# A two-layer MLP behind a per-head tap filter: the order of the prologue on VectorE and ScalarE, the taps, the first loads and the fillers between the turns

## The reference

```
# x (2, 4096, 192), weight_gen (2, 4096, 8 heads, 7 taps), all float32
w = exp(weight_gen - max over taps);  w = w / (sum over taps + 1e-9)
x1[s] = sum over k of w[s, head, k] * x_pad[s + k]        # 6 zero rows ahead of the sequence
x2 = relu(x1 @ w_in) ** 2 @ w_out                         # 192 -> 2048 -> 192
h  = x2 @ w_in2;  out = (h * clip(h + 3, 0, 6) / 6) @ w_out2
```

## Time and profile before

| what | value |
|---|---|
| median of the runs shown | 1148.89 us (1148.46 to 1148.95, 3 runs) |
| the profiled execution's own time | 1147.57 us |
| its span | 1145.8 us |
| busy in the span: TensorE, VectorE, ScalarE | 1128.2, 911.6, 667.6 us |
| TensorE waits for the three turns' taps | 9.4 us |
| mean granted clock of TensorE | 0.995 of full |

### The profile page before, as it was taken

One profiled execution on the slowest core, in us unless ns is written; L12 is line 12 of the kernel. 1 busy time (PEld: TensorE's weight loads), 2 busy tenths in 40 slices (PEclk: granted clock), 3 DMA queues, 4 the chain that ended last, 5 costly groups with the idle time before them and its releaser, 6 DMA issues.

```text
span 1145.8 us, 25809 instructions
## 1 busy us (share of the span) xinstructions
PE 1128.2 (98%) x10046; PEld 1058.5 (92%) x10046; DVE 911.6 (80%) x1005; ACT 667.6 (58%) x741; POOL 3.1 (0%) x10
## 2 busy tenths in 40 slices
PE   9889999999999999999999999999999999999998
PEld 8779899999999999999999999999999999999997
DVE  6768888796987969788796987969788796986665
ACT  5758555556556564655556565564555656565554
POOL 1000000000000000000000000000000000000000
PEclk9989999999999999999999999999999999999999
DMA  7302102002020110202002020110302002010011
GB/s 203 80 2 74 35 6 69 12 14 62 4 73 6 52 28 0 76 4 68 12 9 67 4 72 7 43 37 0 76 4 67 13 3 72 0 38 4 1 16 28
DMA packets 79303, 41.29 MB, mean 36 GB/s; under 512 B 56172, under 2 KB 72300, under 8 KB 79272
## 3 DMA queue, kind: packets, MB, share of 16 engines
q1 hardware_dynamic: 79272, 40.86, 13.8%
HBM read 29.42 MB, written 11.40 MB: 36 GB/s over the span
## 4 chain that ended last, share of the span: by engine, by line
PE 94%; DVE 2%; ACT 2%; issue 1%; DMA 0%; SPq 0%; DVEq 0%; ACTq 0%
PE h_ps L965 44%; PE y_ps L976 29%; PE y_ps L985 20%; DVE acc L620 1%; ACT hid L452 1%; ACT hid L447 1%; ACT hid_hi L460 0%; DVE hid_lo L737 0%; DMA outs<-in_x_dram 0%; DVE prod L635 0%; PE y_ps L954 0%; PE h_ps L915 0%; PE h_ps L944 0%; DVE hid L728 0%; PE y_ps L1070 0%
## 5 line engine op out<-in xcount | busy, mean ns | idle before, releaser
L965 PE MATMUL h_ps<-xt,win 64*128 64x512 f32 (+1 forms) x4644 | 1070.5, 384 | 0.0
L965 PEld LDWEIGHTS h_ps<-xt,win 64*128 64x128 f32 x4644 | 844.8, 185 | 30.4 <-DVE wout L703 0.7
L976 PE MATMUL y_ps<-hid_hi,wout 64*128 64x512 f32 (+1 forms) x2064 | 547.0, 384 | 1.4 <-DVE xt L711 1.4
L463 ACT ACTIVATE hid_hi<-hid 128x1024 fp32r<-128x1024 f32 (+1 forms) x242 | 255.2, 1054 | 334.2 <-DVE hid L728 161.0
L737 DVE TENSOR_TENSOR hid_lo<-hid,hid_hi 128x1024 fp32r<-128x1024 f32 (+1 forms) x258 | 311.2, 1206 | 161.0 <-ACT hid_hi L463 142.4
L976 PEld LDWEIGHTS y_ps<-hid_hi,wout 64*128 64x128 f32 x2064 | 377.7, 185 | 15.5 <-DVE xt L711 2.1
L985 PE MATMUL y_ps<-hid_lo,wout 64*128 64x512 f32 (+1 forms) x1032 | 313.7, 384 | 0.0
L985 PE MATMUL y_ps<-hid_hi,wout 64*128 64x512 f32 (+1 forms) x1032 | 313.7, 384 | 0.0
L976 PE MATMUL y_ps<-hid_lo,wout 64*128 64x512 f32 (+1 forms) x1032 | 313.6, 384 | 0.0
L985 PEld LDWEIGHTS y_ps<-hid_hi,wout 64*128 64x128 f32 x1032 | 189.7, 185 | 6.9
L985 PEld LDWEIGHTS y_ps<-hid_lo,wout 64*128 64x128 f32 x1032 | 189.7, 185 | 6.8
(11 more groups left out here) (88 smaller groups left out, 333.6 us busy)
## 6 DMA issues: line engine op xcount, KB each, us to landing
xwin<-in_x_dram SPq DMA_DIRECT2D x14, 960.0 KB, 5.7
by_feature<-stage SPq DMA_DIRECT2D x52, 96.0 KB, 2.0
out_dram<-outs SPq DMA_DIRECT2D x240, 16.0 KB, 1.5
out_dram<-outs SPq DMA_DIRECT2D x240, 8.0 KB, 1.4
stage<-by_feature SPq DMA_DIRECT2D x13, 256.0 KB, 3.1
stage<-in_moe_w_out_dram SPq DMA_DIRECT2D x8, 384.0 KB, 4.8
stage<-in_moe_w_in_dram SPq DMA_DIRECT2D x8, 256.0 KB, 3.8
stage<-in_moe_w_in_dram SPq DMA_DIRECT2D x16, 128.0 KB, 3.3
```

The lines of the kernel that those rows point to most:

```text
L463: act.activation(hi, hid[:, slot, :, 0:width], ACT.Copy).then_inc(hi_done, 1)
L965: return pe.matmul(h_ps[:, s % 2, t, 0:tokens.stop - tokens.start], win[layer][r, wn, cols], src[r, xn, tokens], start=bool(rows) and n in ...
L976: return pe.matmul(ps[:, 0, tokens], wout[layer][r, tile, w_cols], src, start=bool(rows) and s == 0 and n == 0 and half != 1, stop=not row ...
```

## The change

It writes the prologue's order anew; the loop is untouched.

- SP issues only the near rows of the last 15 partitions of each half; ScalarE's queue issues the other near rows (48 partitions each) as its first act.
- TensorE's first matmuls use a square of ones that VectorE sets, instead of the identity from GpSimd: 14 instead of 15. Between the turned products of chunk 0 two matmuls on 64 rows each stand where one on the whole array stood, and 2 instead of 3 close them.
- Taps of chunk 1 and 2 stand a step or more earlier. The half 0 turn stands behind the first body of step 7 instead of ahead of it, and `split_x1` of a half stands in the step before.
- The squares of steps 10 and 11 go from VectorE to ScalarE, that of step 14 from ScalarE to VectorE. Weight piece 5 is copied by ScalarE, piece 10 by VectorE; the pieces are spread anew. For chunk 0 `y_cross` is copied ahead of `y_main`, and VectorE's add needs only the former.
- SP asks for chunk 1's gates and rows after 6 instead of 10 pieces.

```diff
-    OWN_HI = (5, 7)
+    OWN_HI = (7, 10)
-    GATED = range(10, 14)
-    WARM = 15
+    GATED = (12, 13, 14)
+    WARM = 14
+    MOST, FEW = [(1, 49)], [(49, PB)]
@@ SyncE
-            load_halo(HALO // 2, HALO // 2, x_near_loaded)
-            load_halo(0, HALO // 2, x_far_loaded)
-            for n in range(10):
+            load_halo(sp, HALO // 2, HALO // 2, x_near_loaded, FEW)
+            load_halo(sp, 0, HALO // 2, x_far_loaded, MOST + FEW)
+            for n in range(6):
                 load_piece(n)
             sp.wait_ge(exp_done, 1)
             load_gates(1)
             load_rows(J, J, x_second_loaded)
@@ ScalarE
+            load_halo(act, HALO // 2, HALO // 2, x_near_loaded, MOST)
             act.wait_ge(consts_set, 1)
...
-                if g == 7:
-                    split_x1_hi(1, xt[0], y1_ps, 0)
-                if g == 10:
-                    copy_y(0, STEPS, y2_ps)
...
+                if g == 6:
+                    split_x1_hi(1, xt[0], y1_ps, 0)
...
+                if g == 9:
+                    copy_y(0, STEPS, y2_ps)
@@ VectorE
+            dve.memset(ones, 1.0).then_inc(ones_set, 1)
...
-                dve.wait_ge(y_copied, 2 * c + 2)
+                dve.wait_ge(y_copied, 2 * c + (1 if cross_first(c) else 2))
@@ TensorE
-            def identities(count):
+            def multiply(square, count):
+
                 for n in range(count):
-                    pe.matmul(h_ps[:, 0, 0, 0:P], ident[:, :], ident[:, :], start=True, stop=True)
+                    pe.matmul(h_ps[:, 0, 0, 0:P], square, square, start=True, stop=True)
+
+            def fill():
+                for bank, r in enumerate(ROWS_OF):
+                    pe.matmul(h_ps[:, bank, 0, 0:P], ident[r, :], ident[r, :], start=True, stop=True, tile_position=(r.start, 0))
...
+            pe.wait_ge(ones_set, 1)
+            multiply(ones, WARM)
             pe.wait_ge(ident_ready, 2)
-            identities(WARM)
             for m in range(TAPS):
                 turn_product(m)
                 if m >= 2:
-                    identities(1)
-            identities(3)
+                    fill()
+            multiply(ident[:, :], 2)
...
-                if g == STEPS - 1:
-                    pe.wait_ge(prep_done, prep_value(1, f"add{TAPS - 1}", 0))
-                    turn_att(1, y1_ps, 0)
                 if g == STEPS + SPLIT - 1:
                     pe.wait_ge(prep_done, prep_value(1, f"add{TAPS - 1}", 1))
+                    pe.wait_ge(y_copied, 2)
                     pe.wait_ge(y_added, 1)
                     turn_att(1, y2_ps, 1)
...
                 first_body(g, inn, late, g >= SECOND + 2)
+                if g == STEPS - 1:
+                    pe.wait_ge(prep_done, prep_value(1, f"add{TAPS - 1}", 0))
+                    turn_att(1, y1_ps, 0)
```

More of the change, by code:

```diff
@@ L157, in conv_mlp_kernel @@
         products = [acc[:, :], prod[:, 0, :], prod[:, 1, :], free_hid[:, 0:J * D], free_hid[:, J * D:2 * J * D]]
+        ones = y_main[:, 0:P]
         ident = sb("ident", [P, P])
@@ L283, in gated_value, with cross_first @@
         def gated_value(g):
-            if isinstance(g, int) and g < GATED.stop:
-                return g + 1 - GATED.start
+            if isinstance(g, int) and g < SECOND:
+                return sum(n <= g for n in GATED)
             return g + 1 - (SECOND - len(GATED))
+        def cross_first(c):
+            return isinstance(c, int) and c == 0
         def narrow(g):
@@ L293, in squared_value, with load_halo @@
         def squared_value(g):
-            return g + 1 if g < GATED.start else g + 1 - len(GATED)
+            return g + 1 - gated_value(g)
         block = ctx.enter_context(nc.Block())
+        def load_halo(engine, row, rows, loaded, groups):
+            for start, stop in groups:
+                for b in range(B):
+                    source = bass.AP(x.tensor, ((b * PB + start) * ROWS + row - HALO) * D,
+                                     [[ROWS * D, stop - start], [1, rows * D]])
+                    engine.dma_start(xwin_first[b * PB + start:b * PB + stop, row * D:(row + rows) * D], source).then_inc(loaded, 16)
         @block.sync
@@ L306, in load_piece @@
                     sp.dma_start(dst, src).then_inc(piece_loaded[n], 16)
-            def load_halo(row, rows, loaded):
-                for start, stop in ((1, EVEN), (EVEN, PB)):
-                    for b in range(B):
-                        source = bass.AP(x.tensor, ((b * PB + start) * ROWS + row - HALO) * D,
-                                         [[ROWS * D, stop - start], [1, rows * D]])
-                        sp.dma_start(xwin_first[b * PB + start:b * PB + stop, row * D:(row + rows) * D], source).then_inc(loaded, 16)
             def load_rows(row, rows, loaded):
@@ L383, in _ @@
             load_rows(J, J, x_second_loaded)
-            for n in range(10, PIECES + 3):
+            for n in range(6, PIECES + 1):
                 load_piece(n)
@@ L388, in _ @@
             load_window(2)
-            for n in range(PIECES + 3, 2 * PIECES - 1):
+            for n in range(PIECES + 1, 2 * PIECES):
                 load_piece(n)
@@ L489, in copy_y @@
                     act.wait_ge(x2_lo, 2 * c)
-                act.activation(y_main[:, :], ps[:, 0, :], ACT.Copy).then_inc(y_copied, 1)
-                act.activation(y_cross[:, :], ps[REST:P, 1, :], ACT.Copy).then_inc(y_copied, 1)
+                parts = [(y_main, ps[:, 0, :]), (y_cross, ps[REST:P, 1, :])]
+                for dst, src in parts[::-1] if cross_first(c) else parts:
+                    act.activation(dst[:, :], src, ACT.Copy).then_inc(y_copied, 1)
             def split_x2_main_hi(c, dst):
@@ L555, in _ @@
             exponentials(0)
-            for n in range(3):
+            for n in range(4):
                 split_piece(n)
             split_x1_hi(0, xt[1], y1_ps)
-            for n in range(3, 5):
+            for n in (4, 5):
                 split_piece(n)
             for g in range(SECOND):
-                if g == 7:
-                    split_x1_hi(1, xt[0], y1_ps, 0)
-                if g == 11:
+                if g == 10:
                     split_x1_hi(1, xt[0], y2_ps, 1)
-                if g == 10:
-                    copy_y(0, STEPS, y2_ps)
                 relu(g, 0, g % 2, narrow(g))
-                if g == 2:
+                if g == 1:
                     exponentials(1)
@@ L804, in _ @@
                 weight_lo(n)
-            weight_hi(5)
             for g in range(SECOND):
-                if g in (7, 11):
-                    split_x1_lo(1, xt[0], (y1_ps, y2_ps)[g // 11], g // 11)
-                if g == 10:
-                    add_y(0, y2_ps)
                 if g in GATED:
-                    gate(g, 0, g % 2, HALF)
+                    gate(g, 0, g % 2, narrow(g))
                 if g == 0:
+                    softmax_shift(1)
                     weight_lo(5)
@@ L817, in _ @@
                     weight_hi(7)
+                    softmax_norm(1)
+                if g == 2:
                     weight_lo(7)
-                if g == 2:
-                    softmax_shift(1)
+                    taps(1, [0, 1], 0)
                 if g == 3:
-                    softmax_norm(1)
-                    taps(1, [0, 1, 2], 0)
+                    taps(1, [2, 3], 0)
                 if g == 4:
```

84 lines of the change are left out of this document (39 added, 45 removed).

## The result

| | before | after |
|---|---|---|
| median of the runs (4 each) | 1148.68 us | 1131.76 us |
| lowest to highest | 1147.14 to 1148.95 | 1131.66 to 1132.01 |
| profiled execution, its span | 1147.57, 1145.8 | 1131.66, 1129.9 |

The ratio is 0.9856, with a 95% interval of 0.9839 to 0.9873: 16.9 us less, where 15.0 (and 1133.9 us) were forecast. The kernel after is also much steadier: its four runs lie within 0.35 us, those of before within 1.8.

The account below looks back on a forecast made before the run. TensorE was taken as the bound, its losses in the first 130 us passing unchanged to the end. Terms 4.2 + 6.6 + 3.6 - 0.2 + 0.8 = 15.0 us gave 1132.6, plus 1.3 for the median 1133.9 us; range 1132.0 to 1138.4.

Parts of the forecast that it names:

- First turn: Step 7: waits for the tap sum (2.75), the split (1.05) and a low weight half (0.4) go; 4.2 us gained.
- Second turn: Step 11: wait falls from 4.65 to 0.3 us, split wait 0.37 and half clock 1.9 go; 6.6 us gained.
- Third turn: Step 26: the 2.04 us wait and 1.6 of half clock go, 0.2 taken off for step 21's low half.
- Start: Four edits ahead of step 2, -0.2 + 0.7 + 0.3: 0.8 us gained, bounds -0.5 and 1.3.
- (a): Start, near rows issued earlier but sharing DMA engines with the own rows: 0.2 us later, bounds 0.2 gained, 0.95 lost.
- (b): Start, fillers on 64 rows between turned products: TensorE keeps up with VectorE, turns end 0.6 to 0.8 us earlier.
- (c): Start, closing fillers after the turned products: one fewer makes it 0.27 us earlier.
- From the profiled execution to the median: Last step of the sum: 1.3 us added to the forecast execution of 1132.6, giving a median of 1133.9 us.
- the second turn stays late: Rival: taps before step 11's turn end 1.5 to 2.5 us later, clock falls again; 3.5 to 4.5 us more; chance 0.15.
- The clock falls in the start: Rival: pause, gaps and smaller fillers drop TensorE's clock up to first_sums; 2.5 to 6 us more; chance 0.14.
- Slower: Rival: the clock, once down in the start, stays down; 37 us of half clock would give 1151.2; chance 0.02.
- The waits move: Rival: VectorE is late whatever the order, so less than 2 us is gained, 1146.6 to 1148.9; chance 0.03.

Follow-up runs that it names:

- e1_turn_ahead: The change with the first turn (step 7) put back between the head and the first body, taps still early: 1133.21 us against the change's 1131.76.
- e5_busy_waits: The kernel before, with identity matmuls filling TensorE's waits for the second and third turn: 1146.86 us against 1148.30 for before.
- e8_y_late: The change with the copies of y and the add of y_rest put back behind step 9's high and low halves: 1132.59 us against 1131.76.
- e7_third_late: The change with chunk 2's taps put back to about the steps where they stood before: 1135.97 us against 1131.76.
- e9_late_issue: The change with ScalarE's issue of the near rows put behind its first exponential; in the trace it moved only from 0.75 to 0.89 us: 1131.32 us against 1131.76.
- e10_no_warmup: The change with 1 instead of 14 matmuls of the ones at the start: 1132.66 us against 1131.76.
- e3_whole_filler: The change with the filler between turned products as one whole-array identity matmul instead of two on 64 rows: 1132.40 us against 1131.76.

## Why the prediction was right, and where its steps were not

The kernel is faster by what the first 130 us lost, TensorE's waits went rather than moved, and the clock no longer falls. By step:

- **First turn, 4.2 forecast, 5.22 measured.** The three waits went as said (2.75, 1.05, and that for the weight half, though the last lay in step 6, ahead of the turn, where the relu of step 6 shows 0.35 for it). From that relu to the one of step 9 4.87 us went, not 3.80. The term was too small because it priced a stop at its idle time alone. A stop costs 0.33 us more at the turn (e1_turn_ahead) and 0.26 at the split, so 0.6 of these 1.07. The other 0.5 are not accounted for.
- **Second turn, 6.6 forecast, 6.00 measured.** The turn starts at 56.28 and waits 0.70 us, not 0.3, so the wait gives 3.95 and not 4.35; the mechanism (`y_rest` comes last) was the one named. From the turn to the relu of step 22 it takes 96.30 - 56.28 = 40.02 us instead of 42.07, so 2.05, where 0.37 for the split and 1.9 for the clock were forecast. The 1.9 was right as a gross price (1.87, e5_busy_waits). e5_busy_waits also shows a danger that the sum did not ask for, that TensorE runs ahead and waits for the split; in the change the split is early, and it does not happen. The last 0.2 us are not accounted for.
- **Third turn, 3.4 forecast, 3.94 measured.** 2.04 + 1.6 + 0.3 for the stop is 3.94. The 0.86 us that e5_busy_waits lost there again are not lost in the change, where the taps are out of the way and VectorE is early. The 0.2 us that I took off for step 21 did not show: TensorE has no wait there in the profile.
- **Start, 0.8 forecast, 0.74 measured,** and this agreement is partly luck. (a) was chosen as a loss by late own rows; what came late were the gates. The first product comes at 6.43 and not 6.09, and yet the last one starts at 11.65 against 11.62, since the 0.22 us wait for the near rows is gone: (a) is 0, not -0.2. (b) and (c) together gave what is left. They brought TensorE's first sums 0.89 us forward (from 14.95 to 14.06), of which the relu of step 0 shows 0.74.
- **From the profiled execution to the median.** This is the one step whose sign was wrong. I added 1.3 us because before's median stands that far above its profiled execution; in the text I named the other case, "they go too, down to 1132.6". That case happened. Before's runs in the later comparisons have mean clocks of 0.993 to 0.996, where the profiled execution has 0.995; 0.001 of the span is 2.3 us at half clock, or 1.1 us of time. And e5_busy_waits shows a fall at the first wait for 1.53 us in one execution, in code which the kernel before shares and whose profiled execution kept the clock there. That the slower executions of before are those with this fall is likely, but no trace shows it. The change has no wait over 0.7 us between the start and its last store, its median is within 0.1 us of its profiled execution, and its clock is 0.999 to 1.000. 1132.6 less the 0.9 us by which the terms fell short is 1131.7, the result. The two errors, 0.9 and 1.3 us, point the same way; that the terms themselves came within 0.9 is in part luck, as +1.0 and +0.5 at the first and third turn and -0.6 at the second make it up.

Of the rivals, "the second turn stays late" named the right place but did not come: the wait is 0.70 us, and e8_y_late, which brings back part of it, costs 0.83 us, its wait of 1.22 us leaving the clock at full. "The clock falls in the start" did not come, and "Slower" did not either. "The waits move" is refuted by the table of waits, and e7_third_late shows the opposite way that a late turn is what costs.

The best of all kernels is e9_late_issue at 1131.32 us, 0.44 below the change. Its range of 1131.18 to 1131.77 touches the change's, and its profiled execution, the slowest of its four, is no faster than the change's at any relu compared (step 0 at 17.45 against 17.36), so the gain is small at best, and its cause is not shown.

## What to carry to other kernels

Where one engine is the bound, look for the few places where it waits, move their producers earlier by a step, and put a price on each stop that is higher than the idle time shown: the clock behind it, and 0.3 us of lost overlap. When a clock loss or a wait goes, ask what the bound engine will arrive at too early; here nearly half of the clock's price was lost again at the next wait (e5_busy_waits), unless the next result was early too. And compare two executions between the same two rows rather than from end to end: in several of these kernels a few tenths of a us that looked like the edit's lay in the landing of the first transfers. If a kernel's runs spread, ask whether the change removes the cause of the spread before you add the distance between profiled run and median.

## What the hardware showed that I had not expected

- A wait of 2.75 us left the clock at full in one execution (1.00 in 44 to 46 us of before), and at the same place a wait of 2.79 us dropped it to half in another (0.50 in 44 to 46 us of e5_busy_waits). The fall cost 1.53 us.
- Turns with fillers on 64 rows each raised the clock to full within 6 us of the first of them, after 5.6 us of idling (e10_no_warmup; by the durations, 1.09 and 0.67 us for 16 transposes, while the granted clock read 1.00 throughout).
- A stop of TensorE costs some 0.3 us beyond the idle time shown: 0.33 at the first turn, 0.26 at the split behind it.
- A transfer of 112 KB at the head of one queue landed 1.00 us later (first use at 3.82 against 2.82) when 216 KB were issued from another queue at the same time.
- Two matmuls on 64 rows each, side by side, cost at most 0.32 us; one on the whole array cost 0.42 and made the turned product beside it 0.09 longer (e3_whole_filler).
